# A two-layer expert block on one core: 64-row tiles for the last rows of x, and TensorE's order in blocks of two pairs

## The reference

```python
w = softmax(weight_gen)                                 # batch, seq, 8 heads, 7 taps
x = einsum('bshk,bskhg->bshg', w, windows_of(x, 7))     # 8192 tokens x 192
x = relu(x @ moe_w_in) ** 2 @ moe_w_out                 # 192 -> 2048 -> 192  ("RELU2")
h = x @ moe2_w_in                                       # 192 -> 2048
out = (h * sigmoid(1.702 * h)) @ moe2_w_out             # 2048 -> 192         ("GELU")
```

## Time and profile before

| | us |
|---|---|
| median of 3 runs (1256.33 to 1257.18) | 1256.75 |
| profiled execution, first to last instruction | 1255.6 |
| TensorE matmul busy | 1207.4 |
| VectorE busy | 831.9 |
| ScalarE busy | 615.6 |
| GpSimd busy | 479.6 |

### The profile page before, as it was taken

One profiled execution on the slowest core, in us unless ns is written; L12 is line 12 of the kernel. 1 busy time (PEld: TensorE's weight loads), 2 busy tenths in 40 slices (PEclk: granted clock), 3 DMA queues, 4 the chain that ended last, 5 costly groups with the idle time before them and its releaser, 6 DMA issues.

```text
span 1255.6 us, 15052 instructions
## 1 busy us (share of the span) xinstructions
PE 1207.4 (96%) x5456; PEld 1000.5 (80%) x5456; DVE 831.9 (66%) x706; ACT 615.6 (49%) x616; POOL 479.6 (38%) x249
## 2 busy tenths in 40 slices
PE   1679999999999999999999999999999999999998
PEld 1568888888888888888888888888888888888886
DVE  5888757576675766657576675857667586664553
ACT  1456454545545454454545545454554545445443
POOL 6856408062360905317071450806226080530000
PEclk9899999999999999999999999999999999999999
DMA  6230010010101001010010101001010100100000
GB/s 189 64 116 2 1 44 0 0 44 0 44 0 44 0 0 44 0 44 0 8 36 0 44 0 44 0 0 44 0 44 0 41 3 0 44 0 13 1 11 15
DMA packets 10493, 30.77 MB, mean 25 GB/s; under 512 B 882, under 2 KB 5106, under 8 KB 10352
## 3 DMA queue, kind: packets, MB, share of 16 engines
q1 hardware_dynamic: 10480, 30.60, 7.6%
HBM read 24.30 MB, written 6.29 MB: 24 GB/s over the span
## 4 chain that ended last, share of the span: by engine, by line
PE 93%; DVE 3%; POOL 1%; issue 1%; ACT 1%; DMA 1%; SPq 0%; POOLq 0%; ACTq 0%
PE hidden L611 45%; PE acc L623 9%; PE acc L627 9%; PE acc L625 9%; PE acc L624 9%; PE acc L626 9%; PE hidden L667 1%; DVE g_hi L526 1%; DMA window<-x 1%; DVE g_lo L533 1%; PE hidden L665 1%; PE hidden L656 1%; PE hidden L658 1%; POOL attn L293 1%; POOL term L270 0%
## 5 line engine op out<-in xcount | busy, mean ns | idle before, releaser
L611 PE MATMUL hidden<-xin,win 128*128 128x512 f32 x2560 | 627.5, 392 | 6.9 <-DVE xin L543 6.6
L611 PEld LDWEIGHTS hidden<-xin,win 128*128 128x128 f32 x2560 | 480.2, 189 | 106.5 <-DVE xin L543 4.3
L533 DVE TENSOR_TENSOR g_lo<-gate,g_hi 128x1024 fp32r<-128x1024 f32 x256 | 428.3, 1673 | 149.4 <-ACT g_hi L422 145.0
L413 ACT ACTIVATE first<-hidden 128x1024 f32<-128x1024 f32 x256 | 263.1, 1028 | 356.6 <-PE hidden L611 355.3
L526 DVE CAST g_hi<-gate 128x1024 fp32r<-128x1024 f32 x128 | 137.0, 1071 | 191.2 <-PE acc L627 185.7
L270 POOL TENSOR_TENSOR attn<-window,probs 128x768 f32<-128x768 f32 (+1 forms) x16 | 24.2, 1512 | 602.7 <-DVE probs L513 596.9
L422 ACT ACTIVATE g_hi<-gate 128x1024 fp32r<-128x1024 f32 x128 | 135.8, 1061 | 203.6 <-DVE gate L530 203.6
L270 POOL TENSOR_TENSOR term<-window,probs 128x768 f32<-128x768 f32 (+1 forms) x96 | 209.8, 2192 | 10.4 <-POOL attn L293 9.8
L623 PE MATMUL acc<-g_hi,wout 128*128 128x512 f32 x512 | 200.6, 392 | 12.0 <-DVE g_lo L533 12.0
L627 PE MATMUL acc<-g_lo,wout 128*128 128x512 f32 x512 | 200.0, 391 | 0.0
L624 PE MATMUL acc<-g_lo,wout 128*128 128x512 f32 x512 | 200.0, 391 | 0.0
(11 more groups left out here) (53 smaller groups left out, 383.6 us busy)
## 6 DMA issues: line engine op xcount, KB each, us to landing
window<-x SPq DMA_DIRECT2D x14, 960.0 KB, 5.0
out<-work SPq DMA_DIRECT2D x16, 384.0 KB, 2.5
work<-moe_w_out SPq DMA_DIRECT2D x8, 384.0 KB, 3.4
work<-moe_w_in SPq DMA_DIRECT2D x4, 512.0 KB, 7.1
work<-moe_w_in SPq DMA_DIRECT2D x8, 256.0 KB, 4.2
probs<-weight_gen SPq DMA_DIRECT2D x1, 1568.0 KB, 15.4
window<-x SPq DMA_DIRECT2D x2, 384.0 KB, 12.4
window<-x SPq DMA_DIRECT2D x2, 283.5 KB
```

The lines of the kernel that those rows point to most:

```text
L413: nc.scalar.activation(first[:, s.k, :], hidden_of(s), func, scale=scale).then_inc(first_done, 1)
L533: nc.vector.tensor_tensor(g_lo[:, s.k, :], gate[:, s.k, :], g_hi[:, s.k, :], ALU.subtract).then_inc(g_ready, 1)
L611: last = nc.tensor.matmul(hidden[:, s.slot, c, :], w[:, wi, cols], xt[:, xi, :], start=m == 0, stop=m == len(parts) - 1)
```

## The change

It has two parts.

The low rest of the weight for the remaining rows is no longer a matmul of 128 rows in which these 64 rows stand twice. The rest of a pair's two chunks is put into one tile `tail`, chunk 0 in partitions 0 to 63 and chunk 1 in partitions 64 to 127, and each is multiplied by the high part of x alone, in a matmul of 64 rows (`halves`). The product of the two low rests is left out. For the second half the high part of x must also lie in partitions 64 to 127: a new tile row `X_TWIN`, which ACT copies once per group and layer (at `xT` and at `split`), with semaphores `x1_twin` and `x2_twin`. DVE's and GpSimd's split of such a weight piece becomes two instructions on 64 partitions each.

TensorE's order is made of blocks: the first products of an even and of the following odd pair, then two output products. The even pair ends with its two half matmuls, the odd one begins with them, so four stand together. Behind `xT` and `oT` both output products that were due come after the transposition. `oT` moves one pair later in the list, and in the opening the second `xT` does.

```diff
 def before_round(i):
-    return [other("oT", i - 1), pair(i + 1, FIRST_N + 16 * i - 1, 1, 3, RELU2)]
+    return [pair(i + 1, FIRST_N + 16 * i - 1, 1, 3, RELU2), other("oT", i - 1)]
 ...
 a_round:
-    steps += [other("take", i, after=n + 11), pair(i + 2, n + 14, 0, 2, RELU2)]
-    steps += [other("oT", i), pair(i + 2, n + 15, 1, 3, RELU2)]
+    steps += [other("take", i, after=n + 11)]
+    steps += [pair(i + 2, n + 14 + p, p % 2, p + 2, RELU2) for p in range(2)]
+    steps += [other("oT", i)]
 ...
 split_piece_lo (kind "rest"):
+                for c, rows in enumerate((slice(0, HALF), slice(HALF, P))):
+                    eng.tensor_tensor(tail[layer][rows, 4 * part:4 * part + 4, :], raw[rows, :, c, :],
+                                      hi[rows, :, c, :], ALU.subtract).then_inc(done, 1)
 ...
 ACT, xT:
+                    nc.scalar.activation(xin[s.x][HALF:P, X_TWIN, :], hidden[HALF:P, s.slot, 1, :],
+                                         ACT.Copy).then_inc(x1_twin, 1)
 ACT, split:
+                    act.wait_ge(rest_done, s.g + 1)
+                    nc.scalar.activation(xin[s.x][HALF:P, X_TWIN, :], rest,
+                                         ACT.Copy).then_inc(x2_twin, 1)
 DVE, xT, between L542 and L543:
+                    dve.wait_ge(x1_twin, s.g + 1)
 ...
 hidden_product:
-                    parts = ((W_HI, X_HI), (W_HI, X_LO), (W_LO, X_HI), (W_REST_HI, X_REST),
-                             (W_REST_LO, X_REST))
+                split_first = s.k == 1
+                def whole():
+                    parts = ((W_HI, X_HI), (W_HI, X_LO), (W_LO, X_HI), (W_REST_HI, X_REST))
 ...
+                def halves():
+                    for c, (rows, xi) in enumerate(((slice(0, HALF), X_REST), (slice(HALF, P), X_TWIN))):
+                        last = nc.tensor.matmul(hidden[:, s.slot, c, :], tail[s.layer][rows, s.j, :],
+                                                xt[rows, xi, :], start=split_first, stop=not split_first)
+                    return last
+                if split_first:
+                    halves()
+                    last = whole()
+                else:
+                    whole()
+                    last = halves()
 ...
 run:
-                        if len(behind) > 2:
-                            follow(behind.pop(0), opened)
+                    after = mine[at + 1].what if at + 1 < len(mine) else None
+                    due = s.what != "pair" or s.k == 1 and after not in ("xT", "oT")
+                    while due and len(behind) > 2:
+                        follow(behind.pop(0), opened)
```

## The result

| | before | after |
|---|---|---|
| median of the runs, us | 1256.61 (4 runs, 1256.33 to 1257.18) | 1360.99 (4 runs, 1358.87 to 1362.92) |
| profiled span, us | 1255.6 | 1361.1 |
| one round, from one `xT` to the next, us | 74.65 | 81.16 (81.14 to 81.22) |

The changed kernel is slower: its time is 1.083 of the time before, 95% interval 1.0815 to 1.0846. The forecast was 1320 us with a range to 1352, so the direction was right and the size was not: +104 us instead of +63.

A forecast was written before the change was run, and what follows sets the result against it. TensorE, busy throughout the rounds, was taken as the bound. Waits of 5.9 us less 1.8 saved gave +4.1 a round, +57 over 14; with +2.9 at entry and +3.3 closing, span 1318.8, median 1320 us, range 1294 to 1352.

The forecast's parts named there:

- (b): TensorE's wait for the gate of pair n+7, in front of the first product of n+8: 1.5 us per round.
- (c): TensorE's wait for `x1_ready`, in front of the halves of pair n+9: 1.5 us per round.
- entry of the rounds: Once, ScalarE's copy of `split` delays `first` of pair 11: +2.2 us, and the first `xT` some 0.7 more.
- (a): TensorE's wait in front of `xT` for VectorE's chain to the gate of pair n+6: 2.9 us per round.
- the opening: Before the rounds, the chain to pair 8's `x1_ready` starts behind pair 5's output, equally long: no change, +-3 us.
- The region of halves: Four halves per block, side by side, one exposed load per edge: 0.68 us against 0.91, saving 1.82 per round.
- The bound that I had named for that: Four halves side by side, each edge also waiting for the array to empty and its load: 1.00 us per block.
- rival 1: Halves no cheaper than full matmuls, or edges drain: 1339, 1346 or 1384 us by region size; chance 0.33.
- elsewhere in a round the blocks are harmless: Away from `xT`, `g_ready` is due over 3 us late enough, counted without GpSimd: no wait.
- rival 3: Region of 0.45 us and short waits, VectorE and GpSimd no longer slowing each other before `xT`: 1232 us; chance 0.06.
- Closing: After the rounds, 24 pairs save 2.7 us, against waits at three places and the last two output products: +3.3.
- Rival 2: Region of halves 0.45 us, no edge loss: about 1303 us; counted within the forecast's own 0.57 chance.

The follow-up runs named there:

- order_only: The kernel before, with its ten full matmuls of first product per pair, put in the new block order: 1352.29 us, 1.0761 of before.
- few_taps: The changed kernel with GpSimd's attention in the rounds summing three of seven taps (leaves work out): 1321.64 us, 1.0518 of before.
- nine_blocks: The kernel before with nine full matmuls of first product per pair, not ten (leaves work out), in the block order: 1326.35 us, ratio 1.0554.
- same_rows: The changed kernel with both halves of a pair on rows 0 to 63 (wrong operands for the second): 1390.29 us, 1.1062 of before.
- old_opening: The changed kernel with the second `xT` of the opening behind pair 6 again, not pair 7: 1355.26 us, 1.0782 of before.

## Why the prediction was right and wrong

**Direction: right. Mechanism: right in the main.** The forecast was that the waits around `xT` outweigh what the halves save, and `order_only` shows it by itself. (b) and (c) were forecast as 1.5 and 1.5 and are 1.5 and 1.5, at the places named. At the entry of the rounds TensorE was to wait 2.2 us for `first` of pair 11; the trace has 2.27 of idle time there, 2.4 against the pace. Three steps failed: the size of the edge, VectorE's chain in (a), and the opening.

**The region of halves: a mis-sized term.** I took 0.45 + 2 x 0.11 = 0.68, with an exposed load as the whole price of an edge. It is 0.89: the load also begins only 0.09 after the turn of the matmul ahead, so an edge costs 0.20 to 0.22. The bound that I had named for that, 1.00 with 0.165 for the array to empty, was nearer. It is 1.7 us per round, 24 us in all; by my own formula 16 of them reach the total, as (a) and (c) shrink when TensorE comes later.

By the Trainium skill ("TensorEngine Tiling (Array Packing)", Key Properties), a change of the tiling mode drains TensorE. The trace agrees with it in part: the load for the halves is held back past the last full matmul's turn, but it starts at 602.99, while that matmul's record ends at 603.06, and an edge costs 0.20 to 0.22 and not the 0.27 of my bound. I had it as a part of rival 1, which had 0.33 in all, and not as the forecast.

**Wait (a): VectorE's chain was counted too short.** Forecast 2.9, and by my own formula 2.5 with the true region; measured 3.5, which is 14 us more in 14 rounds. From the end of pair n's output product (616.92) to `xT` the chain takes 19.3 us, where I had 18.35. VectorE was counted with 4.12 us for a RELU2 pair beside GpSimd. In the changed kernel, where output products come in twos, VectorE has both pairs at hand and works back to back:

```profile
610.16 2.75 DVE L562 TENSOR_TENSOR g_lo<-gate,g_hi 128x1024 fp32r<-128x1024 f32 x1
612.83 2.03 DVE L555 CAST g_hi<-gate 128x1024 fp32r<-128x1024 f32 x1
614.90 2.75 DVE L562 TENSOR_TENSOR g_lo<-gate,g_hi 128x1024 fp32r<-128x1024 f32 x1
617.57 2.03 DVE L555 CAST g_hi<-gate 128x1024 fp32r<-128x1024 f32 x1
```

That is 4.74 a pair, since `g_hi` takes 2.03 instead of 1.42: 1.2 us more over two pairs. It also begins 0.4 late, for VectorE is still at pair n+1 when my time zero comes. That is the wait for `g_lo` of pair n+1, 0.9 us, and it contradicts my line that elsewhere in a round the blocks are harmless: I had counted that slack without GpSimd. The GELU pairs behind took 0.7 less than counted, since the second had 3.6 and not 4.30. The sign was in the rows of before: the `g_lo` of two pairs start at 645.04 and 649.78, 4.74 apart, and I had left the idle time between them out.

`few_taps` shows that this takes GpSimd's work. It also bears out rival 3's price for (a) without contention, 0.9 us, or 0.45 with the true region: 0.5 are left. (Its working "7.2 + 0.26" has the 0.26 twice; 7.24 - 6.35 gives the 0.9.)

**Opening: a term I set to nothing.** I compared the chain `g_hi`, `g_lo`, L542, L543 and left out that VectorE does one pair more and the softmax step ahead of the second `xT`'s operands. 7.3 us are lost up to the first round where I had 2.9: pair 8 starts 4.0 later, its stretch loses 0.9 more to the clock (2.6 us at a granted clock of 0.61, against 1.7 at 0.73 before), and the entry costs 2.4. **Closing:** 105.5 - 7.3 - 14 x 6.5 = 7.2 against 3.3 forecast; it holds the same kinds of wait and region, and was not tested apart.

Sum of the misses: 14 x (6.5 - 4.1) = 34, opening 4, closing 4: the 42 us between 1318.8 and the span of 1361.1.

**The expectation of a ceiling.** Rival 2 said that lossless halves give 1303 us; `nine_blocks` is that case without ScalarE's copies and took 1326. Its rounds lose 4.1 us each where rival 2 had 2.9, 17 of the 23 us; the rest is outside the rounds.

## What to carry to other kernels

Where TensorE is busy all the time, changing between full and half-row tiles has a price per change, here 0.20 to 0.22 us: four halves that save two matmuls (0.45 us) just pay for two changes. Count the changes, not the matmuls.

Grouping an engine's work in larger blocks takes away slack at the single places where something else (here a transposition) takes a buffer's turn. Follow for each such place the chain from the last release to the next need; and when a chain is counted beside a busy neighbour engine, take the distance from one start to the next, or durations from work that is back to back, not the durations of work with gaps.

## What the runs showed of the hardware

Two 64-row matmuls on different rows into different PSUM banks start together: 0.23 us per couple, where two couples on the same rows cost 0.47 us more (`same_rows`). What I had not expected is that VectorE and GpSimd fall into one period. In the changed kernel GpSimd's two instructions of a tap begin 4.73 us after those of the tap before, and VectorE's `g_hi` and `g_lo` stretch to the same 4.74 us:

```profile
612.00 2.31 POOL L291 TENSOR_TENSOR term<-window,probs 128x768 f32<-128x768 f32 x1 [0.17 <-POOL attn L314]
614.28 2.29 POOL L314 TENSOR_TENSOR attn<-attn,term 128x768 f32<-128x768 f32 x1
616.74 2.31 POOL L291 TENSOR_TENSOR term<-window,probs 128x768 f32<-128x768 f32 x1 [0.17 <-POOL attn L314]
```

Before, GpSimd had the same period of 4.73 us. VectorE's held 0.54 and then 0.33 us of idle time, and its `g_hi` took 1.42 and 1.62: the shorter the gap, the longer the `g_hi`, and the sum stayed. Why it does so no run here shows.

In the rounds the new waits, up to 1.3 us of idle time each, left the granted clock at 1.00 (149.28 to 1204.42). In the opening it fell behind idle times of 7.84 us (0.61), of 3.90 us before (0.73), and of 2.81 us in `old_opening` (0.72), though before it had stayed at 1.00 behind 2.93 us. So the length of one idle time alone does not tell whether it falls, and the prediction's bar for adding nothing rested on one such case.
